# A tile of its own for M6+M1, tokens prepared one pair ahead, parts split last, and two raw buffers, in an attention and feed-forward kernel

## What is computed

```python
qn = q / (norm(q, axis=1) + 1e-6);  kn = k / (norm(k, axis=1) + 1e-6)
a = softmax(kn.T @ qn / tau)          # 256 x 256 per batch
x = (v @ a).reshape(B * N, C)
h = x @ w_in;  g = h * sigmoid(h)     # SiLU
out = g @ w_out
```

## Time and profile before

| what | value |
|---|---|
| median of 3 runs | 1188.86 us (1186.72 to 1191.2) |
| the profiled execution | 1185.15 us, of it 1183.3 us from first to last instruction |
| PE, PEld busy | 90%, 73% |
| DVE, ACT busy | 79%, 77% |
| POOL busy | 25% |
| mean granted TensorE clock | 0.963 of full speed |

### The profile page before, as it was taken

How to read it: one execution, slowest core, us unless ns; L and a number is a source line. 1 busy time by engine, 2 the same in 40 slices (tenths; PEclk the granted TensorE clock), 3 DMA queues, 4 the chain that set the end, 5 groups by cost and what they waited for, 6 DMA issues and landing times.

```text
span 1183.3 us, 15134 instructions
## 1 busy us (share of the span) xinstructions
...
## 2 busy tenths in 40 slices
...
GB/s 361 397 255 15 235 89 72 211 207 162 156 163 173 151 160 166 150 154 179 140 186 153 179 175 118 183 172 143 168 170 145 168 170 147 156 170 108 142 119 92
DMA packets 107841, 197.06 MB, mean 167 GB/s; under 512 B 9424, under 2 KB 42320, under 8 KB 107632
## 3 DMA queue, kind: packets, MB, share of 16 engines
...
...
HBM read 145.82 MB, written 50.23 MB: 166 GB/s over the span
## 4 chain that ended last, share of the span: by engine, by line
PE 50%; ACT 15%; DMA 13%; DVE 10%; issue 8%; SPq 1%; POOL 1%; DVEq 0%; ACTq 0%; POOLq 0%
PE ps_h L802 9%; DMA out_t_dram<-o_sb 8%; PE ps_h L803 8%; PE ps_h L804 8%; PE ps_o L860 5%; PE ps_o L861 5%; PE ps_o L862 5%; PE ps_h L860 3%; PE ps_h L862 3%; PE ps_h L861 3%; ACT ps_h L1043 3%; ACT gx_hi L1203 2%; ACT h L1159 2%; DVE g_lo L1546 2%; ACT w L1151 2%
## 5 line engine op out<-in xcount | busy, mean ns | idle before, releaser
L1546 DVE TENSOR_TENSOR g_lo<-h,g_hi 128x512 fp32r<-128x512 f32 (+1 forms) x296 | 204.0, 692 | 39.2 <-ACT g_hi L1182 36.6
L802 PE MATMUL ps_h<-b_hi,a_hi_mid 128*128 128x512 f32 (+1 forms) x336 | 141.4, 421 | 60.2 <-ACT h L1159 53.2
...
L1182 ACT ACTIVATE g_hi<-h 128x512 fp32r<-128x512 f32 (+1 forms) x296 | 182.5, 620 | 10.5 <-PE ps_h L862 3.8
L803 PE MATMUL ps_h<-b_lo,a_hi_mid 128*128 128x512 f32 (+1 forms) x336 | 136.0, 405 | 0.0
L804 PE MATMUL ps_h<-b_hi,a_lo_mid 128*128 128x512 f32 (+1 forms) x336 | 135.3, 403 | 0.0
L802 PEld LDWEIGHTS ps_h<-b_hi,a_hi_mid 128*128 128x128 f32 x336 | 67.1, 200 | 90.5 <-ACT h L1159 58.9
L860 PE MATMUL ps_h<-g_hi,ring 128*128 128x512 f32 (+1 forms) x264 | 103.6, 393 | 13.3 <-DVE h L1541 6.1
L1580 DVE TENSOR_TENSOR gx_lo<-t_raw,gx_hi 128x1024 fp32r<-128x1024 f32 (+1 forms) x88 | 107.0, 1216 | 1.0 <-ACT gx_hi L1189 0.9
L1558 DVE TENSOR_TENSOR t_raw<-h 128x1024 f32<-128x1024 f32 (+1 forms) x88 | 105.3, 1196 | 0.0
L860 PE MATMUL ps_o<-gx_hi,ring 128*128 128x512 f32 (+1 forms) x264 | 102.7, 389 | 0.7 <-DVE gx_lo L1590 0.4
L862 PE MATMUL ps_h<-g_hi,ring 128*128 128x512 f32 (+1 forms) x264 | 102.9, 390 | 0.0
...
## 6 DMA issues: line engine op xcount, KB each, us to landing
...
ring<-s_dram SPq DMA_DIRECT2D x88, 256.0 KB, 3.2
out_t_dram<-fl_sb POOLq DMA_DIRECT2D x72, 256.0 KB, 5.8
x_raw<-v_t_dram SPq DMA_DIRECT2D x58, 256.0 KB, 4.0
x_raw<-v_t_dram POOLq DMA_DIRECT2D x45, 256.0 KB, 6.5
out_t_dram<-o_sb POOLq DMA_DIRECT2D x36, 256.0 KB, 5.2
out_t_dram<-o_sb SPq DMA_DIRECT2D x27, 256.0 KB, 2.7
...
```

The lines of the kernel that those rows point to most:

```text
L802: nc.tensor.matmul(out, w_hi, x_hi, start=start, stop=False, skip_group_check=True)
L803: nc.tensor.matmul(out, w_hi, x_lo, start=False, stop=False, skip_group_check=True)
L1182: nc.scalar.activation(g_hi[:, g, 0:tok], h[:, g, 0:tok], ACT.Copy).then_inc(hi[g], 1)
L1546: nc.vector.tensor_tensor(g_lo[:, g, 0:tok], h[:, g, 0:tok], g_hi[:, g, 0:tok].bitcast(F32), ALU.subtract).then_inc(lo[g], 1)
```

## The change

- `u_sum` is a new tile; `sum_u` writes into it and waits for `o1_copied`, `c21_stored` and `nv_made` of earlier work in place of `o1_stored`. `add_u` and `make_nv` read it.
- From step 2 on the accumulating token DMAs are issued in pairs 0, 1 and 5 instead of 2, 3 and 6, `load_x` stands behind `load_ring_b`, and the rounding of T2, T1, T3 and T4 is one pair earlier. `sum_c22` and `store_c22` go from pair 4 to 5. TensorE waits for T4's split only at `p4`.
- In step 0 `split_part`, one part per pair from pair 1 on, and `split_x` stand at the end of VectorE's pair, `round_x` behind `copy_w` on ScalarE; the tokens of step 1 are loaded ahead of the first parts. In the turning pair `split_part` stands last.
- `w_out` parts 1 to 3 are rounded by GpSimd (`round_wo`) instead of ScalarE; the table for SiLU is loaded by a tiny activation ahead.
- `a1_raw` and the sums of batch two's factors get two buffers each, and the reloads other pairs.
- The last block C12 is stored by ScalarE's queue instead of GpSimd's.

The diff, cut to what the prediction speaks of:

```diff
+        u_sum = sb("u_sum_sb", [P, TOK])
+        a1_raw1 = sb("a1_raw1", [P, 4, P])
+        sums1 = sb("sums1", [P, 4, P])
...
-        reload_at = {SWITCH + max(2 * pair - 1, 0): pair for pair in range(PAIRS)}
+        reload_at = {SWITCH + 1 + 3 * pair // 2 + pair // 6: pair for pair in range(PAIRS)}
...
             def load_a1(pair):
                 sp.wait_ge(a_split, PAIRS)
-                if pair:
-                    sp.wait_ge(a1_split, pair)
-                sp.dma_start(a1_raw[:], a1_dram[:, pair]).then_inc(a1_loaded, 16)
+                if pair >= 2:
+                    sp.wait_ge(a1_split, pair - 1)
+                sp.dma_start(a1_raw[pair % 2][:], a1_dram[:, pair]).then_inc(a1_loaded[pair % 2], 16)
...
+            sp.wait_ge(v_split, 3)
+            load_x(1)
             sp.wait_ge(wp_summed, 2 * FOLDS)
             load_part(0)
             load_part(1)
-            sp.wait_ge(v_split, 3)
-            load_x(1)
...
-                if pair == PAIRS - 1 and it + 2 < ALL:
-                    sp.wait_ge(x_split, 3 + FACTORS * it)
-                    load_x(it + 2)
                 load_ring_b(n)
                 if n + 1 in reload_at:
                     load_a1(reload_at[n + 1])
+                if pair == PAIRS - 1 and it + 2 < ALL:
+                    sp.wait_ge(x_split, x_groups(it + 1))
+                    load_x(it + 2)
...
+            def round_wo(n):
+                pool.wait_ge(wo_loaded[n], 16)
+                pool.wait_ge(chunk_scored, PLACE[SPLIT[-1]] + 1)
+                nc.gpsimd.tensor_copy(wo_part(wo_hi, n), wo_part(wo_raw, n)).then_inc(wo_rounded_pool, 1)
...
+            for n in range(1, PARTS):
+                round_wo(n)
             add_x_first(1)
...
-                if pair == 2 and it + 1 < ALL:
+                if pair == (0 if it > 1 else 2) and it + 1 < ALL:
                     add_x_first(it + 1)
-                if pair == 3 and it + 1 < ALL:
+                if pair == (1 if it > 1 else 3) and it + 1 < ALL:
                     add_x_second(it + 1)
-                if pair == 6 and it + 1 < ALL:
+                if pair == (5 if it > 1 else 6) and it + 1 < ALL:
                     add_x_third(it + 1)
...
-            ROUND_X = {2: (B11, B21), 3: (B22,), 4: (T2,), 5: (T1,), 6: (T3,), 7: (T4,)}
+            ROUND_X_SECOND = {2: (B11, B21), 3: (B22,), 4: (T2, T1), 5: (T3,), 7: (T4,)}
+            ROUND_X = {2: (B11, B21), 3: (T2, B22), 4: (T1,), 5: (T3,), 6: (T4,)}
...
-            SPLIT_X_FIRST = {4: (T1, T3), 5: (B11, B22), 7: (T4, T4)}
-            SPLIT_X = {3: (B11,), 4: (B21,), 5: (B22, T2), 6: (T1, T3), 7: (T4,)}
+            SPLIT_X_FIRST = {3: (T1, T2), 4: (T3, T3), 6: (B11, B22), 7: (T4, T4)}
+            SPLIT_X_SECOND = {3: (B11, B21), 4: (B22,), 5: (T2, T1), 6: (T3,)}
+            SPLIT_X = {3: (B11,), 4: (B21, T2), 5: (B22,), 6: (T1, T3), 7: (T4,)}
...
             def sum_u(it):
                 tok = tokens_of(it)[1]
                 dve.wait_ge(used_t2, PAIRS * it)
-                dve.wait_ge(o1_stored, 16 * it)
-                nc.vector.tensor_tensor(o1[:, 0:tok], m6[:, 0:tok], o1[:, 0:tok], ALU.add).then_inc(u_summed, 1)
+                dve.wait_ge(o1_copied, it)
+                if it > 1:
+                    dve.wait_ge(c21_stored, 32 * (it - 1))
+                    dve.wait_ge(nv_made, it - 1)
+                nc.vector.tensor_tensor(u_sum[:, 0:tok], m6[:, 0:tok], o1[:, 0:tok], ALU.add).then_inc(u_summed, 1)
...
-            PARTS_AT = {2: (0, 1), 3: (2,), 4: (3,), 6: (4,), 8: (5,), 10: (6,), 12: (7,)}
+            PARTS_AT = {1: 0, 2: 1, 3: 2, 4: 3, 6: 4, 8: 5, 10: 6, 12: 7}
...
                 split_h(n, TOK, H12)
+                if PAIRS - EARLY - 1 <= n < PAIRS - 1:
+                    split_a(0, n + 1)
                 if n < PAIRS - 2:
                     sum_a(0, n + 2)
+                if n in PARTS_AT:
+                    split_part(PARTS_AT[n])
+                if n in SPLIT_X_FIRST:
+                    split_x(1, *SPLIT_X_FIRST[n])
```

More of the change, by code:

```diff
@@ L277, in channel_attention_ffn @@
         used_t4 = sem("used_t4")
-        part_loaded = sem("part_loaded")
+        part_loaded = [sem(f"part_loaded{n}") for n in range(2)]
         part_step = sem("part_step")
@@ L285, in channel_attention_ffn @@
         a1_saved = sem("a1_saved")
-        a1_loaded = sem("a1_loaded")
+        a1_loaded = [sem(f"a1_loaded{n}") for n in range(2)]
         a1_step = sem("a1_step")
@@ L345, in width, with x_groups, x_place @@
             return tokens_of(n // PAIRS)[1]
-        reload_at = {SWITCH + max(2 * pair - 1, 0): pair for pair in range(PAIRS)}
+        reload_at = {SWITCH + 1 + 3 * pair // 2 + pair // 6: pair for pair in range(PAIRS)}
+        assert all(SWITCH + pair < n <= SWITCH + PAIRS - 2 + pair for n, pair in reload_at.items())
+        X_FIRST = ((T1, T2), (T3, T3), (B11, B22), (T4, T4))
+        X_SECOND = (B11, B21, B22, T2, T1, T3, T4)
+        X_LATER = (B11, B21, T2, B22, T1, T3, T4)
+        def x_groups(step):
+            return len(X_FIRST) + FACTORS * (step - 1)
+        def x_place(step, block_):
+            if step == 1:
+                return 1 + [block_ in range(a, b + 1) for a, b in X_FIRST].index(True)
+            return x_groups(step - 1) + 1 + (X_SECOND if step == 2 else X_LATER).index(block_)
         def part_tiles(i):
@@ L834, in p4 @@
                 pe.wait_ge(c22_made, n + 1)
+                if pair == 0 and n:
+                    pe.wait_ge(x_split, x_groups(n // PAIRS))
                 product(pair, par, tok, BANK_Y, A22, T4, False).then_inc(p4_done, 1)
@@ L1296, in first_step @@
                 copy_w(n, TOK)
+                if n >= 3 and n - 3 < len(X_FIRST):
+                    round_x(1, *X_FIRST[n - 3])
                 silu_c22(n, TOK)
@@ L1344, in pair_step @@
                 if it < FINAL:
[L1345 removed]
+                    for block_ in (ROUND_X if it > 1 else ROUND_X_SECOND).get(pair, ()):
                         round_x(it + 1, block_, block_)
@@ L1667, in pair_step @@
                     make_nv(it - 1)
-                if it > 1 and pair == 4:
+                if it > 1 and pair == 5:
                     sum_c22(it - 1)
@@ L1679, in pair_step @@
                 make_c21(n, tok)
-                for i in PARTS_AT.get(n, ()):
-                    split_part(i)
+                if it == 1 and pair == PAIRS - 1:
+                    split_x(2, T4, T4)
+                if n in PARTS_AT:
+                    split_part(PARTS_AT[n])
                 if n - 1 in reload_at:
```

117 lines of the change are left out of this document (54 added, 63 removed).

## The result

The changed kernel takes 1091.07 us (median of 4 runs, 1088.67 to 1093.67) against 1188.24 of the kernel before in the same runs: a ratio of 0.918, 95% interval 0.9151 to 0.9209. The forecast was 1081, range 1066 to 1106. Direction and main mechanism came as forecast; the gain was 97 us in place of 107. The profiled execution took 1090.23 us, 1088.4 of it from first to last instruction.

The account below looks back on a forecast made before the run. TensorE's busy time was taken as the floor, with VectorE's waits at sum_u (58.9 us) and for round_x (22.4) above it; terms summed to -107.4 from 1188.86, giving 1081 us, range 1066 to 1106.

Parts of the forecast that it names:

- Wide steps: Seven passes, 2 to 4 and 7 to 10: from 616.6 us to 7 x 78.7 = 550.9, -65.7, mostly pair 2's wait gone.
- The flush: Pair 3 of a wide pass: one more DMA ahead of ScalarE's flush costs 1.15 us, making it 0.4 us late.
- Rival C: The wait moves to the flush: a further 4 us, ScalarE waits 3.3 in pair 3; +35, 1116 us; chance 0.10.
- Step 0: First pass over eight pairs: part splits use VectorE's free time, 100.7 to 90 us, -10.7, bounds -6 and -12.
- Step 5: Pass 5: pair 2 loses ring-load and sum_u waits, 21.7 to 9.8 us; tokens' gain goes; -12, 92.0 to 80.
- Step 6: Pass 6: pair 2 -5.3, pairs 6 and 7 -2.4, reload pairing stays in pair 4; -7.7, bounds -4 and -11.
- step 1: Pass 1: pair 2 still waits for load_x(2), the tokens' pairs gain; 91.1 to 87 us, -4.
- Step 11: Last pass, without tokens and narrow: pair 2 loses its 7.4 us; -7.3.
- Wo: w_out parts rounded by GpSimd: up to -0.85 us in pair 0, about 1 cost beside second softmax's reciprocals; 0.
- B: VectorE takes over as the bound, pairs settling at 10.1 us: +15 in the middle, 1096 us; chance 0.17.
- D: The wait stays: a new condition of sum_u is as late as the old; +74, 1155 us; chance 0.03.
- E: Slower than before: add_x_second on GpSimd holds up pair 2's flush, 12 us lost in nine passes; 1195 us; chance 0.02.

Follow-up runs that it names:

- x_second_late: The changed kernel with add_x_second issued in pair 2 behind that pair's flush, not in pair 1 ahead of it, from step 2 on: 1087.27 us, ratio 0.9146.

## Why the prediction was right, and where it was off

**Wide steps** (forecast -65.7, measured -66.4). Right by its own steps: `sum_u`'s wait gone with no other wait of VectorE in its place, 7.4 us a step, of which 5.7 were wait and 1.7 clock; the tile alone and the tile undone show the same price from both sides. Pairs 4 and 6 are the 10.1 that pair 5 was, as said. The line drawn, 81 us for a wide step, was kept by 1.6 us or more.

**The flush** (forecast 0.4 late in each step, in pair 3). The term is right in kind and in its sum over the wide steps (2.9 us for 2.8), wrong in place: it falls in pair 2, at 0.3 to 1.05 us in four wide steps and nothing in the other three. By the forecast's own sign, a wait over 0.5 us, 0.4 was too small where it did fall: ScalarE waited 0.8 to 1.5 us there. Rival C, priced at 35, is real at a tenth of that. Its pricing was by DMAs "in front" at (8.1 - 5.8) / 2 = 1.15 us each; the two flushes of step 5 issued at 538.1 and 545.0 and landing 1.5 us apart say that it is the finish of the DMAs in front that counts.

**Step 0** (forecast -10.7, measured -5.0). The step that failed is "1.3 for small waits that stay". The working followed the parts and the tokens but not `split_a(0, 6)` and `split_a(0, 7)`, which the diff moves from ahead of `make_c22` to the end of VectorE's pair: their price was not written down at all. It is 3.9 to 5.7 us, and with it undone the step takes 90.07, the 90 of the forecast. Of what pairs 2 and 3 gained, over half came with something else than the place of the part splits, probably the order of the loads, which the forecast named but gave no size.

**Step 5** (forecast -12, measured -2.6). The 21.7 us pair did fall, to 11.5. The step that failed is "Three reloads instead of two fall among its pairs 4 to 7, so its tokens' gain goes": it gave the reloads' GpSimd work no price of its own, though the earlier trace rows had a pair of 13.6 us for it, and the term was sized as 80. The arithmetic on GpSimd costs 9.1 us in that step, by the run without it, and 6 to 12 against the other lengths the step had. In the kernel before, the long wait of pair 2 hid part of this, as two runs show: with the tile alone pair 2 of step 5 lost 6.0 us and pairs 3 to 5 took 4.6 more, and with the tile undone pair 2 took 5.3 more and pairs 3 and 4 gave back 3.3. The forecast took pair 2's wait off and left its neighbours as they were. The length of step 5 is also the least certain of all: 86.3 to 92.2 us in the traces of seven kernels with the same work in it (two of them with one token DMA a pair later).

Here a rule can be held against the trace. VectorE's addition into `t_raw`, 896 columns, both inputs in SBUF, in the changed kernel and in x_second_late, each beside GpSimd's additions:

```profile
546.43 3.11 DVE L1584 TENSOR_TENSOR t_raw<-h 128x896 f32<-128x896 f32 x1
548.02 0.55 POOL L691 TENSOR_TENSOR sums<-sums,a_raw 128x128 f32<-128x128 f32 x1
548.65 1.19 POOL L693 TENSOR_TENSOR sums<-sums,a_raw 128x128 f32<-128x128 f32 x1
```

```profile
547.65 1.33 DVE L1584 TENSOR_TENSOR t_raw<-h 128x896 f32<-128x896 f32 x1
547.94 1.35 POOL L686 TENSOR_TENSOR sums<-a_raw 128x128 f32<-128x128 f32 x1
```

It takes 1.09 us with GpSimd idle. The Trainium skill ("SBUF — State Buffer", Who interferes with whom) says that such an instruction contends with one of GpSimd that reads SBUF and that the shared pair is an exclusive lock. The 3.11 us agrees: GpSimd's additions stood end to end from 546.18 to 548.57, the last four of them at their own 0.55 to 0.57 us, and only the next one, at 548.65, was held up, to 1.19; VectorE's 1.09 us of work, counted back from its end at 549.54, begin at 548.45. In the other trace VectorE's addition came first, by 0.29 us; it is only 0.24 us longer than alone, and GpSimd's took 1.35 in place of 0.55. So in these two traces the engine that came second waited. That this is what moves step 5 by 6 us from trace to trace is likely, but not shown.

**Step 6** (-7.7, measured -7.3) and **step 1** (-4, measured -3.4) are right in their sums, with some luck. In step 6 pair 2 lost 4.8 us and pairs 6 and 7 2.4, as said; but the 13.6 us pair, which was to stay in pair 4, is 11.6 there, and pair 1 takes 11.7 where it took 10.2, which was not forecast. In step 1 pairs 6 and 7 lost 3.0 us, and pair 2 still waited for its tokens, as said, but took 14.9 us and not "some 17"; pairs 1 and 3 took 1.8 more. In the traces of the other kernels with this step 1 it took 87.2 to 90.0 us. Step 6 without GpSimd's arithmetic takes 83.8: its cost is not that but, by VectorE's 77.1 busy us there against 70.8 in step 2, the seven or eight more instructions of the reload; this is read from the windows, no run isolates it.

**Step 11** gave 9.1 for 7.3. Pair 2 gave its 7.5; the rest is the end, which was put at 0: the last pair with what follows it takes 21.8 us in both kernels that store C12 by GpSimd's queue and 20.0 to 20.1 in the twelve that store it by ScalarE's. **Wo** gave 0 for 0, but by another way: the forecast set 1 us of cost against 0.85 of gain, and neither was seen. Of its two readings the one by which "the reciprocals would cost nothing" held. The 1.2 us ahead of step 0 are less than the scatter: step 0 starts at 98.3 to 100.8 in the traces of kernels that are alike up to there.

**Rivals.** B (VectorE takes over) was weighed by a wrong reading: 63.7 us of step 2 is the busy time of PEld in the earlier trace rows; VectorE's is 71.05, so in 78.7 us it had some 8 us free and not 15. It does not hold in the wide steps all the same (VectorE busy 70.8 of 79.3, pairs at the forecast's values), so the margin was half of what the forecast took it for. It does hold in the reload pairs, where it was not looked for. D and E were not seen; E's 12 us in nine steps would also give 1189 and not 1195. The sum of the steps missed by 12.4 us: steps 5, 0, 1 and 6 were put 9.4, 5.7, 0.6 and 0.4 too low, the wide steps, step 11 and the front 0.7, 1.8 and 1.2 too high. The time missed by 10, as the median after stands 2.7 us over its span where 5.6 was carried over from before, and 0.5 was rounded away.
